# A paired start for a delta-rule recurrence fused with two MLPs: 64-token units of all four batches, and seven MLP steps ahead of unit 2

## The reference

```python
# B, H, S, D = 4, 8, 768, 40
for t in range(S):
    y[:, :, t] = einsum('bhd,bhde->bhe', r_t, state)
    Sa = einsum('bhde,bhe->bhd', state, a_t)
    state = state * w_t[:, :, None, :] - einsum('bhd,bhe->bhde', Sa, b_t) + einsum('bhd,bhe->bhde', v_t, k_t)
x = y.transpose(0, 2, 1, 3).reshape(3072, 320)
h = x @ w_in;  x = maximum(0.01 * h, h) @ w_out            # 320 -> 2048 -> 320
x = sigmoid(x @ w_gate) * (x @ w_val) @ w_out2             # 320 -> 1536 -> 320
```

## Time and profile before

| | |
|---|---|
| median of 3 runs | 1150.48 us (1150.15 to 1153.25) |
| the profiled execution | 1145.99 us, span 1144.3 us |
| PE busy | 1043.0 us (91%) |
| DVE busy | 595.5 us (52%) |
| ACT, POOL busy | 397.3 us (35%), 106.1 us (9%) |
| mean granted clock | 0.962 |
| chain that ended last | PE 77%, DVE 10%, issue 6%, DMA 3% |

### The profile page before, as it was taken

One profiled execution on the slowest core, in us unless ns is written; L12 is line 12 of the kernel. 1 busy time (PEld: TensorE's weight loads), 2 busy tenths in 40 slices (PEclk: granted clock), 3 DMA queues, 4 the chain that ended last, 5 costly groups with the idle time before them and its releaser, 6 DMA issues.

```text
span 1144.3 us, 35947 instructions
## 1 busy us (share of the span) xinstructions
PE 1043.0 (91%) x15840; PEld 890.5 (78%) x15840; DVE 595.5 (52%) x1306; ACT 397.3 (35%) x782; POOL 106.1 (9%) x99
## 2 busy tenths in 40 slices
PE   2366859999999999999999999999999999999998
PEld 1355758887878777777788887888888888888887
DVE  6697867668676866667655224443223232323222
ACT  2141433434434534444343335542223222222222
POOL 7022020202020110101000000000000000000000
PEclk9985559999999999999999999999999999999999
DMA  5737263445436352634243033220200102010000
GB/s 185 211 119 219 60 175 75 125 99 153 110 112 159 94 152 51 174 86 140 48 137 87 18 96 115 106 88 1 60 1 23 38 1 60 1 60 1 23 1 23
DMA packets 134985, 99.79 MB, mean 87 GB/s; under 512 B 96560, under 2 KB 111920, under 8 KB 134832
## 3 DMA queue, kind: packets, MB, share of 16 engines
q1 hardware_dynamic: 132384, 85.06, 27.5%
q0 software_dynamic: 2448, 12.45, 3.0%
HBM read 78.61 MB, written 18.87 MB: 85 GB/s over the span
## 4 chain that ended last, share of the span: by engine, by line
PE 77%; DVE 10%; issue 6%; DMA 3%; ACT 2%; POOL 1%; SPq 1%; ACTq 0%; DVEq 0%; POOLq 0%
PE bank L736 14%; PE bank L787 11%; PE pair L787 11%; DVE prod L1150 4%; DVE t_unit L1154 4%; PE bank L807 4%; PE bank L805 4%; PE bank L806 4%; PE bank L751 4%; PE bank L752 3%; PE bank L753 3%; PE bank L712 2%; PE bank L755 2%; PE bank L703 2%; PE bank L756 2%
## 5 line engine op out<-in xcount | busy, mean ns | idle before, releaser
L1199 DVE TENSOR_TENSOR g_lo<-g_full,g_hi 128x512 fp32r<-128x512 f32 x168 | 121.6, 724 | 232.9 <-ACT g_hi L969 232.8
L969 ACT CAST g_hi<-g_full 128x512 fp32r<-128x512 f32 x168 | 104.4, 621 | 134.7 <-DVE g_full L1251 131.6
L736 PE MATMUL bank<-x_hi,w_up 128*128 128x512 f32 x480 | 134.6, 410 | 2.1 <-ACT x_hi L978 2.1
L962 ACT ACTIVATE g_full<-bank 128x512 f32<-128x512 f32 x96 | 57.4, 598 | 214.4 <-PE bank L736 201.7
L1150 DVE TENSOR_TENSOR prod<-t_unit,p_unit 128x126 f32<-128x126 f32 (+22 forms) x372 | 107.4, 289 | 35.7 <-DMA p_unit<-p_dram 24.5
L1154 DVE TENSOR_TENSOR t_unit<-t_unit,prod 128x126 f32<-128x126 f32 (+22 forms) x372 | 107.3, 288 | 12.8
L736 PEld LDWEIGHTS bank<-x_hi,w_up 128*128 128x128 f32 x480 | 85.4, 189 | 21.2 <-ACT x_hi L978 2.5
L1251 DVE TENSOR_TENSOR g_full<-pair,h_sb 128x512 f32<-128x512 f32 x36 | 24.9, 692 | 112.8 <-PE pair L787 112.1
L736 PE MATMUL bank<-x_lo,w_up 128*128 128x512 f32 x288 | 81.7, 392 | 0.0
L559 PE MATMUL bank<-a_sb,b_sb 40*64 40x64 f32 x768 | 34.9, 254 | 50.5 <-POOL a_sb L290 37.3
L751 PE MATMUL bank<-g_hi,w_dn 128*128 128x512 f32 x192 | 76.7, 399 | 4.6 <-DVE g_lo L1199 4.5
(11 more groups left out here) (141 smaller groups left out, 2328.9 us busy)
## 6 DMA issues: line engine op xcount, KB each, us to landing
b_sb<-in_bF SPq DMA_DIRECT2D x12, 512.0 KB, 5.9
a_sb<-in_aF SPq DMA_DIRECT2D x24, 256.0 KB, 6.2
k_sb<-in_kF SPq DMA_DIRECT2D x12, 512.0 KB, 4.4
p_unit<-p_dram SPq DMA_DIRECT2D x24, 256.0 KB, 3.9
v_sb<-in_vF SPq DMA_DIRECT2D x12, 512.0 KB, 6.6
r_sb<-in_rF SPq DMA_DIRECT2D x12, 512.0 KB, 8.2
w_raw<-in_wF SPq DMA_DIRECT2D x20, 260.0 KB, 3.7
stage<-in_w_out POOLq DMA_DIRECT2D x7, 640.0 KB, 4.3
```

The costliest lines, as they stand in the source:

```text
L736: last = nc.tensor.matmul(up_bank(m)[:], lhs, rhs, start=(e == 0), stop=(e == len(products) - 1))
L969: nc.scalar.copy(g_hi[:, m % 2], g_full[:]).then_inc(g_hi_ready, 1)
L1199: nc.vector.tensor_tensor(g_lo[:, m % 2], g_full[:], g_hi[:, m % 2].bitcast(F32), ALU.subtract).then_inc(g_lo_ready, 1)
```

## The change

A unit is now 64 tokens of all four batches: c is the batch pair, and half units 2u and 2u+1 do not depend on each other. Only the host layouts and the place that `store_y` writes to say so. Each state waits for that of two half units before (`state_ready` n-1 instead of n, and st_sb by c).

For units 0 and 1 every engine has a new list (`tensor_start`, `scalar_start`, `vector_start`, the heads of the POOL and SP programs), in which both half units go through each group one behind the other. To let them, the odd half units of these two units get second copies of the small tiles, in memory of weights that come later (spare_a, spare_b, spare_c), and use banks 0 to 3, which the MLP does not yet need. Unit 1 has its own p_unit and t_unit in spare_b, so that its inverse can start right behind that of unit 0. The combined `pe_a_ka` takes "a" and "ka" apart in the start.

The MLP starts in slot 0 of window 2, in front of unit 2:

```diff
-        def mlp_step(g, s):
+        STEPS = {(2, 0): [0, 1, 2, 3, 4, 5, 6], (2, 1): [7], (2, 2): [], (2, 3): [8], (2, 4): [], (2, 5): [],
+                 (2, 6): [9], (2, 7): [], (3, 0): [10], (3, 1): [], (3, 2): [11], (3, 3): [], (3, 4): [12], (3, 5): [],
+                 (3, 6): [13], (3, 7): []}
+
+        def mlp_steps(g, s):
+            if (g, s) in STEPS:
+                return STEPS[g, s]
             m = 8 * g + s - LAG
-            return m if 0 <= m < M1 else None
+            return [m] if 0 <= m < M1 else []
...
+        def tensor_start(pe):
...
+            pe_rhs_begin(pe, 0)
+            pe_rhs_begin(pe, 1)
+            pe_rhs_end(pe, 0)
+            pe_rhs_end(pe, 1)
+            pe_sn(pe, 0)
+            pe_sn(pe, 1)
+            pe_a_ka(pe, None, 2)
+            pe_a_ka(pe, None, 3)
...
+        def vector_start(dve):
+            for n in range(4):
+                dve_decay(dve, n)
+            dve_ka(dve, 0)
+            dve_ka(dve, 1)
+            dve_decay(dve, 4)
+            inverse_first(dve, 0)
+            inverse_columns(dve, 0, 0, C - 1)
+            dve_ka(dve, 2)
+            dve_ka(dve, 3)
+            dve_decay(dve, 5)
+            inverse_first(dve, 1)
+            inverse_columns(dve, 1, 0, C - 1)
+            dve_st(dve, 0)
+            dve_st(dve, 1)
...
+        def vector_first_steps(dve):
+            inverse_first(dve, 2)
+            inverse_columns(dve, 2, 0, 6)
+            dve_g_low(dve, 0)
+            dve_decay(dve, 7)
+            dve_g_low(dve, 1)
+            inverse_columns(dve, 2, 6, 11)
+            dve_g_low(dve, 2)
...
                     if s == 1:
                         if soon:
                             dve_ka(dve, n + 2)
-                        if later and n + 5 >= 4:
+                        if later:
                             dve_decay(dve, n + 5)
+                        if g == START:
+                            inverse_first(dve, g + 1)
+                            inverse_columns(dve, g + 1, 0, 13)
...
-                dst = x1[j, 2 * hf:2 * hf + 2].rearrange("b (q i e) (c t) -> c i e (b q) t", i=2, e=D, c=2)
+                dst = x1[j, 2 * c:2 * c + 2].rearrange("b (q i e) (c t) -> c i e (b q) t", i=2, e=D, c=2)
```

More of the change, by code:

```diff
@@ L1259, in vector_program @@
                 for s in range(8):
-                    m = mlp_step(g, s)
-                    if g == -2 and s == 0:
-                        for first in range(4):
-                            dve_decay(dve, first)
+                    if (g, s) == (START, 0):
+                        vector_first_steps(dve)
+                        continue
                     elif s == 0 and soon:
```

563 lines of the change are left out of this document (403 added, 160 removed), and 9 rows, old and new, of tables (START_BANKS, START_ORDER).

## The result

| | before | after |
|---|---|---|
| median, beside each other | 1151.14 us (1150.15 to 1153.25, 4 runs) | 1172.8 us (1166.13 to 1176.43, 4 runs) |
| the profiled execution | 1145.99 us, span 1144.3 | 1176.43 us, span 1174.7 |
| mean granted clock | 0.962 | 0.956 |

The change makes the kernel **slower: ratio 1.0179, 95% interval 1.0131 to 1.0227**. The prediction of 1145 us (1128 to 1163) is wrong, and so is its sign.

What follows compares the result with a forecast made beforehand. Recurrence and DVE bound the start, PE everything from step 0. Window 4 at 126 + 123 + 3.5 = 252.5 us against 257.9, 5.4 us earlier: 1140.6 us for the profiled execution, 1145 us from the median (range 1128 to 1163).

Steps and rivals of the forecast that it cites:

- last y_sb of block 0, Y: End of block 0's recurrence in the start: ready at 110 us (bounds 104 and 121) against 145.05 before.
- Y to step 0: From block 0's last y_sb to the first MLP step: 16.3 us, with DVE's queued work ahead of x_lo; step 0 at 126.
- step 0 to window 4: From the first MLP step to step 14: 123 us at 2.4 GHz, plus 3.5 us for stretches at 1.2 GHz.
- from window 4 to the end: From step 14 on: same PE work in the same order, so the same distance to the end as before.
- Rival 4: In the start a weight piece or POOL load holds ACT or PE: Y near 125, 1160 us; chance 0.02.
- The clock term in the start: Before Y: y of half unit 1 at 84.5 us, between 80 and 90; unit 1 takes 24.5, nearer the 1.2 GHz end.
- rival 1: The dense start gets the fast clock: Y at 104, window 4 at 241 us, 1134 us in all; chance 0.2.
- The walk: Engine lists followed from step 0 to window 4: 18 to 19 us of PE idle, including 4.6 for t_sb.
- Rival 3: Windows 2 and 3, thin in steps, fall to 1.2 GHz: + 14 us, window 4 at 263, 1156 us; chance 0.3.
- Rival 2: DVE waits behind step 0 eat the gain exactly: window 4 at 256 to 259 us, 1149 to 1152 us; chance 0.2.
- The signs that the prediction named for being wrong: First up later than 135 us, clock below 0.8 before window 4, or the end moving by another amount than step 14.

Runs made afterwards that it cites:

- e3: The changed kernel with weight pieces 0 to 3 loaded after b and a of unit 2, and ACT's splits later; ratio 1.0146.
- e1: The kernel before with only the new units (host layouts, looser state waits), lists and MLP steps kept; 1148.79 us against 1150.75, ratio 0.9994.
- e2: The changed kernel with the MLP steps where they were before, one per slot from slot 2 of window 2; 1172.16 us, ratio 1.0209.
- e8: The changed kernel with e3's edit, DVE and ACT start lists reordered, e7's edit, and g_lo of step 14 ahead of inverse columns; 1157.43 us, ratio 1.0073.
- e9: The changed kernel with k and b of units 5 and 6 ahead of x, and step 14's g_lo ahead of inverse columns; ratio 1.0136.
- e10: e8 with e9's earlier k and b, plus three more orders (unit 3's k, unit 2's columns, columns ahead of y); 1150.29 us against 1147.66, ratio 1.0017.
- e4: The changed kernel with weight pieces 4 to 7 loaded behind k of unit 2; 1170.84 us, ratio 1.0181.
- e7: The changed kernel with the first 13 columns of unit 3's inverse behind st and vrur of half unit 4; 1162.33 us, ratio 1.0143.
- e11: e10 with window 2's ka, state and vrur ahead of the inverse's rest, and window 4's evictions ahead of the wait for x; ratio 1.0035.

## Why the prediction was wrong

Against the forecast for the profiled execution (1140.6 us) the changed kernel is 35.8 us late. By the prediction's own steps:

| step of the prediction | forecast | measured | short by |
|---|---|---|---|
| last y_sb of block 0, Y | 110 (104 to 121) | 123.2 | 13.2 |
| Y to step 0 | 16.3 | 17.6 | 1.3 |
| step 0 to window 4 | 123 + 3.5 | 131.6 | 5.1 |
| from window 4 to the end | as before | +15.9 | 15.9 |

(The rest of 0.3 us is rounding, above all 110 + 16.3 taken as 126.)

- **The start up to Y was the first step that failed.** Up to y of half unit 1 it was 5.4 us late (89.9 against 84.5), for the larger part by the weight pieces: they were costed at nothing, but issued beside the p stores they held back k, DVE and t_sb. e3, without that, has the second inverse and `pe_first` within 1.4 us of the forecast and this y at 86.8. The other 7.8 us lie in unit 1 (33.3 us from there to Y, forecast 25.5), where four stops on late pages of code make 9.5: 3.95, 3.01, 1.45 and 1.08. Rival 4, that a piece of weight or a POOL load holds ACT or PE in the start, put Y near 125 and the time at 1160 us, and got 0.02. Its cause and its Y were near; what the pieces held were small stores and, with the other loads, PE's own code.
- **The clock term in the start was nearly right.** The prediction took y of half unit 1 at 84.5, between 80 at 2.4 GHz and 90 at 1.2, and unit 1 near its slow end. Measured were 0.71 (estimated as above) and 0.62, where the kernel before has 0.63 and 0.58: the pair lists get little more of the fast clock, and rival 1, which gave it to them, was wrong. The 0.76 that it leaned on counts time without a record as full speed. The page TensorE: Matmul & The Clock Gate of the Trainium skill (Part 1) says that activity releases the throttle. The trace agrees in part: the clock rose at 74.61 us in the middle of dense work, but the 11.8 us of it before that, with PE busy all along, were at 1.2 GHz.
- **Y to step 0** was right, by its terms too: PE's wait of 10.0 us for ka behind the splits is the DVE queue that was counted.
- **Step 0 to window 4**: 22.6 us idle (27.4 + 59.3 + 44.9 less 26.7, 42.2 and 40.1 busy) against 18 to 19 forecast, and 109.0 busy against 108. t_sb was forecast at 4.6 and took 5.4, the two waits for POOL 3.9 and 3.9 us. The largest miss is one row: rhs of half unit 5 waited 6.2 us for a bank behind DVE's 13 columns and behind a decay that itself waited 3.2 us for w_raw, where I had y wait 4.0. The walk followed the data and forgot who empties the bank, and the transfer of w_raw.
- **"From step 14 the same distance to the end" failed worst**, 15.9 us of 35.8. It rested on equal lists from window 4 on. But a list runs as before only if its inputs are there as before. Window 3 has four steps instead of eight: y of half unit 7 is evicted fewer steps ahead of window 4, so the stores, x of block 1, k of unit 5 and p_unit that the MLP used to cover lie open. e1 and e2, which keep the eight steps, take 52.2 and 54.8 us for window 4. p_unit came so late that g_lo of step 14, behind it in DVE's queue, held PE for 4.1 us, and the clock fell behind the wait (0.92 in the window). Here are the two rows, on DVE and on PE:

```profile
277.26 0.19 DVE L1402 TENSOR_TENSOR prod<-t_unit,p_unit 128x31 f32<-128x31 f32 x1 [7.65 <-DMA p_unit<-p_dram]
285.27 0.50 PE L883 MATMUL pair_low<-g_hi,w_dn 128*128 128x512 f32 x1 [4.08 <-DVE g_lo L1452]
```

- e8, e9 and e10 take these waits apart one by one: 8.1 us in window 4 become 4.3, not none. The other 7.5 us are those of windows 7 and 8 (57.6 and 58.5 us at a clock of 0.94), and their cause is open. Two stops on late pages fell there, of 1.83 us at 452.8 and 1.63 us at 509.8, and the clock fell right behind each. e2, e3 and e4 lose 5 to 8 us in the two windows as well; but with the same lists there as the changed kernel e7 takes 54.8 and 54.2 us and e9 54.7 and 55.4, so the lists alone don't bring it. Part of the 9 us by which the profiled pair overstates the medians may be this.
- **Rival 3** (thin windows fall to 1.2 GHz, 0.3) was right that they fall: 0.86 and 0.89. But they cost 4.5 us of busy time up to step 14 (109.0 against the 104.5 of the walk at 2.4 GHz), not the 14 of the rival. **Rival 2** had the idle time right and nothing else (DVE's share in the first of its two stretches is 94% by the earlier trace rows, not 96).

The signs that the prediction named for being wrong did show: the first up came later than 135 us, and the end moved by another amount than step 14 (30.4 and 14.5 us).

What can be had at best is not shown. In the best orders tried, e10 and e11, T is 38 us earlier and the way from there to step 14 takes 128 us instead of 90.5, so step 14 comes out at 257.6 and 258.2 us: the start gave back just what was put off. But both still have waits of 5.2 us for t_sb and more.

## What to carry to other kernels

- Work that is moved in front of a bottleneck engine also takes away its cover: the steps taken out of windows 2 and 3 laid open transfers and DVE queues, one window further on as well. Before trusting "the rest is unchanged", ask for the first window behind the change which transfer was issued how many steps ahead, and how many there are now.
- For each wait, follow who empties the bank, not only who makes the data. And mending one wait of a saturated engine (DVE in window 2) moves it: judge by where the next step begins, not by the wait that has gone.
- Keep bulk loads away from stretches with many small matmuls, and behind the small stores of a critical chain: in e3 that alone brought the second inverse 3.6 us forward.
- A mean clock can cover time for which the profile has no record. Check it by the pace of the same matmuls where the clock is on record.
